# Accumulator copies at the block borders of the second MLP moved ahead of the next step's polynomial, and the last three steps' products with g_l taken last

## The chip, the cores and the metric

The kernel runs on one core of one Trainium2 chip. The metric is the device time of one execution in microseconds (us). A core has five engines with queues of their own: TensorE (PE in the profile; PEld are its weight loads), VectorE (DVE), ScalarE (ACT), GpSimd (POOL) and SyncE (SP), which here only issues DMAs. They meet through semaphores: an instruction adds to one when it is done, and another queue waits until it has a count. Each queue runs strictly in its own order, so whatever stands behind a waiting instruction waits too.

## The reference

A linear attention over 4 batches of 768 positions (8 heads of 48) gives 3072 tokens of 384 numbers. Two MLPs with 2048 hidden features follow:

```python
def _moe_ref(x, w_in, w_out):
    h = x @ w_in
    r = np.maximum(h, 0.0)
    return (r * r) @ w_out

def _moe2_ref(x, w_in, w_out):
    h = x @ w_in
    g = h - np.tanh(h)
    return (g @ w_out).astype(np.float32)
```

The change is in the second MLP and in the turn to it from the first.

## The kernel before

**Tiling.** The 3072 tokens are 6 blocks of 512 columns (`BLOCKS`), the 2048 hidden features 16 tiles of 128 (`FT`). A step m is one tile of one block, m = 16 i + f, 96 steps an MLP. For each step TensorE computes a hidden tile of 128 x 512 (`first1`, `first2`) and adds its contribution to three accumulators acc[0], acc[1], acc[2] of 128 x 512 in PSUM (`second1`, `second2`). Each float32 number is split into a rounded high part and a remainder, and each product is three products, high x high, high x low and low x high (`product3`, lines 542 to 544; the traces call the data `_h` and `_l`). So either half of a step is nine matmuls of 512 columns, a step eighteen.

**Order on TensorE.** Hidden tiles run three steps ahead (`LAG = 3`): first2(m + 3), second2(m), first2(m + 4), second2(m + 1), and so on. In the last three steps no hidden tile is left. Hidden tiles lie in four PSUM buffers in turn, named sc and hid in the traces. When a block ends (f = 15), its accumulators must be copied out before second2 of the next block may start again on them: it waits for ScalarE's copies of acc[0] and acc[2] (semaphore s_outa) and VectorE's copy of acc[1] (s_outd), each just ahead of the products that need it.

**From a hidden tile to g.** g = h - tanh(h) is computed with a short polynomial where h is small. For step k, in this order:
- ScalarE squares the tile (`square`, line 424), shifts the square (`shifted`, line 430), and puts the table's tanh into PSUM, tile y (`table_tanh`, line 434).
- POOL multiplies the shifted square by the square (`square_poly`, line 340).
- ScalarE makes the ratio of it (`make_ratio`, line 438).
- VectorE in `poly_pick(k)` compares the square with a bound (line 820), multiplies tile and ratio (line 822), picks the table's tanh where the square is large (line 826), and subtracts (line 831), which gives g_f.
- ScalarE rounds g_f to g_h (`hi2`, line 445), and POOL takes the remainder g_l (`lo2`, line 345). second2(k) waits for g_l.

ScalarE's order for a step is that of `step2(k)`: square(k), shifted(k), table_tanh(k), hi2(k-1), make_ratio(k). POOL's is square_poly(k), lo2(k-1). At a block border (m = 16 i + 15, k = m + 3) the copies come in: on ScalarE acc[0] and acc[2] around table_tanh(k), with the copies on line 463, and on VectorE acc[1] (`keep_out`, line 840) behind poly_pick(k). SyncE stores each copied accumulator to the output (line 297), three stores of 256 KB a block, the last three at the very end.

**The turn between the MLPs.** The first three hidden tiles of the second MLP and their step2 run in the last three steps of the first. The first MLP's last accumulators are copied by `keep_x2(5)`: on ScalarE lines 417 and 419, behind step2(2); on VectorE line 767, ahead of poly_pick(2). Behind its copies ScalarE converts the last unit of the second MLP's weights (`split_hi`, line 392), and POOL takes that unit's remainder (`split_lo`, line 335) ahead of square_poly(3). `split_x2` (ScalarE line 455, VectorE line 835) splits the next block's input in steps 4 to 6 of each block.

Of the kernel before, what the change touches and what calls it, by code (L numbers as in the profile page):

```python
# [9 lines left out]
ACT = mybir.ActivationFunctionType  # L10
AX_X = mybir.AxisListType.X

P = 128
# [3 lines left out]
KC, FT = C // P, FF // P  # L17
# [7 lines left out]
STEPS = BLOCKS * FT  # L25
LAG = 3
# [13 lines left out]
def build(nc, tt, nat, w_col, u_rep, win1, wout1, win2, wout2, out):  # L40
    with ExitStack() as ctx:
# [11 lines left out]
        wout_h = sb("wout_h", [P, FT, C], F32R)  # L53
        wout_l = sb("wout_l", [P, FT, C], F32R)

        x2T = sb("x2T", [P, BLOCKS, KC, N])
# [4 lines left out]
        g_h = sb("g_h", [P, 4, N], F32R)  # L61
        g_l = sb("g_l", [P, 4, N], F32R)
# [45 lines left out]
        acc = [acc01[:, 0:512], acc01[:, 512:1024], acc2[:, :]]  # L108
# [279 lines left out]
        @block.scalar  # L388
        def _(act):
            def split_hi(mlp, n):  # L390
                act.wait_ge(*landed(mlp, n))
                act.activation(unit_parts(n)[0], unit_raw(mlp, n), ACT.Copy).then_inc(s_whi, 1)

            def diagonal(T):

                act.wait_ge(s_c, T + 1)
                after(act, s_y, T - 1)
                for h in range(H):
                    ins = act.activation(scores[T % 2][:, h % 2, h // 2, :], ident, ACT.Copy,  # L399
                                         scale=c_sum[T % 2][:, h:h + 1])  # L400
                ins.then_inc(s_diag, 1)

            def x_high(T):
                i, j = T // TPB, T % TPB
                act.wait_ge(s_y, T + 1)
                after(act, s_h1, FT * (i - 1))
                act.activation(x_h[:, i % 2, :, P * j:P * j + P],
                               y_ps(T)[:, 0:KC * P].rearrange("p (c t) -> p c t", c=KC), ACT.Copy).then_inc(s_xh, 1)

            def hi1(m):  # L410
                act.wait_ge(s_g1, m + 1)
                after(act, s_o1, m - 3)
                act.activation(g_h[:, m % 4, :], g_f[:, m % 2, :], ACT.Copy).then_inc(s_gh1, 1)  # L413

            def keep_x2(i):
                act.wait_ge(s_acc1, 2 * i + 1)
                act.activation(x2T[:, i, 0, :], acc[0], ACT.Copy).then_inc(s_x2a, 1)
                act.wait_ge(s_o1, FT * i + FT)
                act.activation(x2T[:, i, 2, :], acc[2], ACT.Copy).then_inc(s_x2a, 1)

            def square(m):
                act.wait_ge(s_h2, m + 1)
                after(act, s_sel, m - 1)
                act.activation(sq[m % 2], hid2[m % 4], ACT.Square).then_inc(s_sq, 1)

            def shifted(m):

                act.wait_ge(s_sq, m + 1)
                after(act, s_small, m - 1)
                act.activation(ratio[m % 2], sq[m % 2], ACT.Copy, bias=C3_OVER_C5).then_inc(s_qq, 1)  # L430

            def table_tanh(m):
                after(act, s_sel, m)
                act.activation(tanh_ps[:, :], hid2[m % 4], ACT.Tanh).then_inc(s_tanh, 1)

            def make_ratio(m):
                act.wait_ge(s_pp, m + 1)
                act.activation(ratio[m % 2], ratio[m % 2], ACT.Copy, scale=C5, bias=1.0).then_inc(s_ratio, 1)  # L438

            def hi2(m):  # L440
                act.wait_ge(s_g2, m + 1)
                if m < 4:
                    act.wait_ge(s_o1, STEPS - 3 + m)
                after(act, s_o2, m - 3)
                act.activation(g_h[:, m % 4, :], g_f[:, m % 2, :], ACT.Copy).then_inc(s_gh2, 1)  # L445

            def split_x2(i, c):

                act.wait_ge(s_x2a, 2 * i + 2)
                act.wait_ge(s_x2d, i + 1)  # L450
                if i < 2:
                    act.wait_ge(s_h1, STEPS - FT * (1 - i))
                else:
                    act.wait_ge(s_h2, FT * (i - 1))
                act.activation(x_h[:, i % 2, c, :], x2T[:, i, c, :], ACT.Copy).then_inc(s_x2h, 1)

            def keep_out(i, c):
                if c == 0:
                    act.wait_ge(s_acc2, 2 * i + 1)
                else:  # L460
                    act.wait_ge(s_o2, FT * i + FT)
                after(act, s_x2l, KC * (i + 1))
                act.activation(x2T[:, i, c, :], acc[c], ACT.Copy).then_inc(s_outa, 1)

            act.wait_ge(s_powT, 1)
            act.activation(dec_k, hid34[:, 0:512].rearrange("p (h e) -> p h e", h=H)[:, :, 0:D],
                           ACT.Copy).then_inc(s_tab, 1)
            act.wait_ge(s_const, 3)
            diagonal(0)
            diagonal(1)  # L470
            split_hi(0, 0)
            x_high(0)
            diagonal(2)
            x_high(1)
            diagonal(3)
            x_high(2)
            split_hi(0, 1)
            x_high(3)
            split_hi(0, 2)
            for m in range(LAG):  # L480
                hi1(m)

            def step2(k, ends=None):

                if k < STEPS:
                    square(k)
                    shifted(k)
                if ends is not None:
                    keep_out(ends, 0)
                if k < STEPS:  # L490
                    table_tanh(k)
                if ends is not None:
                    keep_out(ends, 2)
                if k > 0:
                    hi2(k - 1)
                if k < STEPS:
                    make_ratio(k)

            for i in range(BLOCKS):
                for n in range(FT):  # L500
                    m = FT * i + n
                    T = scores_at(i, n)
                    if T is not None:
                        diagonal(T)
                    if m + LAG < STEPS:
                        hi1(m + LAG)
                    T = y_at(i, n)
                    if T is not None:
                        x_high(T)
                    if i == 0 and n in SPLIT1_AT:  # L510
                        split_hi(0, SPLIT1_AT[n])
                    if i == BLOCKS - 1 and n in SPLIT2_AT:
                        u = SPLIT2_AT[n]
                        if u % 2 == 0:
                            act.wait_ge(s_h1, STEPS - FT + 2 * u + Q)
                        else:
                            act.wait_ge(s_o1, STEPS - FT + 2 * (u - 1) + Q)
                        split_hi(1, u)
                    if i == BLOCKS - 1 and n in SPLIT_X2_AT:
                        split_x2(0, SPLIT_X2_AT[n])  # L520
                    if m + LAG >= STEPS:
                        step2(m + LAG - STEPS)
                    if n == FT - 1:
                        keep_x2(i)
            act.wait_ge(s_o1, STEPS)
            split_hi(1, SPLIT2_AT[FT])
            for m in range(STEPS):
                i, n = divmod(m, FT)
                k = m + LAG
                if k <= STEPS:  # L530
                    step2(k, i if n == FT - 1 else None)
                elif n == FT - 1:
                    keep_out(i, 0)
                    keep_out(i, 2)
                if n in SPLIT_X2_AT and i < BLOCKS - 1:
                    split_x2(i + 1, SPLIT_X2_AT[n])

        @block.tensor
        def _(pe):
# [92 lines left out]
            def first2(m):  # L632
# [11 lines left out]
                                  x_h[:, i % 2, c, :], x_l[:, i % 2, c, :], c == 0, c == KC - 1)  # L644
                mm.then_inc(s_h2, 1)

            def second2(m):
                i, f = divmod(m, FT)
                pe.wait_ge(s_gl2, m + 1)
# [46 lines left out]
            for m in range(STEPS):  # L696
                if m + LAG < STEPS:
                    first2(m + LAG)
                second2(m)

        @block.vector
        def _(dve):
# [62 lines left out]
            def keep_x2(i):  # L765
                dve.wait_ge(s_acc1, 2 * i + 2)
                dve.tensor_copy(x2T[:, i, 1, :], acc[1]).then_inc(s_x2d, 1)
# [70 lines left out]
            def keep_out(i):  # L838
                dve.wait_ge(s_acc2, 2 * i + 2)
                dve.tensor_copy(x2T[:, i, 1, :], acc[1]).then_inc(s_outd, 1)  # L840
# [27 lines left out]
                        poly_pick(m + LAG - STEPS)  # L868
            for m in range(STEPS):
                i, n = divmod(m, FT)  # L870
                if m + LAG < STEPS:
                    poly_pick(m + LAG)
                if n in SPLIT_X2_AT and i < BLOCKS - 1:
                    split_x2(i + 1, SPLIT_X2_AT[n])
                if n == FT - 1:
                    keep_out(i)


def feature_order():
# [62 lines left out]
```

## Time and profile before

| | |
|---|---|
| median of 3 runs | 936.95 us (936.81 to 939.05) |
| the profiled execution | 937.0 us, its span 935.2 us |
| TensorE's mean granted clock | 0.983 |
| busy share of the span: PE, PEld, DVE, ACT, POOL | 96%, 79%, 63%, 48%, 51% |
| chain that ended last | PE 80%, DVE 8%, ACT 4%, POOL 3%, issue 3%, DMA 1% |
| turn to the second MLP | about 530 us from the span's start |

Times in the rows count from the start of the span, in us. The profiled execution's time beside its span, 937.0 and 935.2, differs by 1.8 us, which lie around the span. Ends of matmuls are modelled: a matmul's row lasts 0.39 us, while the next one starts 0.227 us later. The granted clock is a share of TensorE's full speed of 2.4 GHz; 0.50 is the lower level, 1.2 GHz. A row's name in brackets is the instruction whose end released it, and the number ahead of it the idle time of the engine before the row.

### The profile page before, as it was taken

To read this page: it belongs to the slowest core of one execution; us is meant where nothing else is said; L and a number is where in the kernel's file an instruction comes from. 1 tells how busy PE (TensorE), PEld (TensorE's weight loads), DVE (VectorE), ACT (ScalarE), POOL (GpSimd) and SP (SyncE) were. 2 spreads that over 40 slices of the span, in tenths; PEclk is the share of its full clock that TensorE was granted. 3 is DMA by queue.
4 is the path that set the end of the run, shared out by engine and by line. 5 is a ranking of instruction groups with operands and counts; after the bars stand their busy time and mean duration, and the time that the engine had idled before them with its cause. 6 is when DMAs were issued, how large, how long until landed. Compare 5 with 4: busy or idle time off the path is not lost.

```text
span 935.2 us, 13868 instructions
## 1 busy us (share of the span) xinstructions
PE 901.3 (96%) x5340; PEld 739.3 (79%) x5340; DVE 589.1 (63%) x789; ACT 453.5 (48%) x852; POOL 479.9 (51%) x370
## 2 busy tenths in 40 slices
PE   5889999999999999999999999999999999999998
PEld 5767888888888888888888788788788788788786
DVE  6368645545554554454356587687687687687675
ACT  3333413222321322232223677677677677677674
POOL 5444344425334432433346777566566566566564
PEclk8799999999999999999999999999999999999999
DMA  6343111210211121120113000000000000000000
GB/s 250 129 180 138 53 52 53 105 53 21 84 53 53 53 105 53 29 78 25 78 61 108 1 1 1 34 1 1 34 0 1 34 1 1 34 1 1 35 0 34
DMA packets 12162, 47.49 MB, mean 51 GB/s; under 512 B 1472, under 2 KB 1600, under 8 KB 12096
## 3 DMA queue, kind: packets, MB, share of 16 engines
q1 hardware_dynamic: 12096, 46.60, 13.6%
q8 instruction: 42, 0.69, 0.3%
q14 instruction: 24, 0.20, 0.1%
HBM read 41.88 MB, written 4.72 MB: 50 GB/s over the span
## 4 chain that ended last, share of the span: by engine, by line
PE 80%; DVE 8%; ACT 4%; issue 3%; POOL 3%; DMA 1%; POOLq 0%; DVEq 0%; ACTq 0%
PE acc L542 13%; PE acc L544 12%; PE acc L543 12%; PE hid L543 9%; PE hid L544 9%; PE hid L542 9%; PE sc L542 3%; PE sc L543 3%; PE sc L544 3%; PE sc L560 3%; PE y L588 2%; PE sc L596 2%; PE y L574 2%; POOL area L340 1%; POOL g_l L345 1%
## 5 line engine op out<-in xcount | busy, mean ns | idle before, releaser
L329 POOL TENSOR_TENSOR g_l<-g_f,g_h 128x512 fp32r<-128x512 f32 x96 | 131.6, 1372 | 277.4 <-ACT g_h L413 277.4
L542 PE MATMUL acc<-g_h,wout_h 128*128 128x512 f32 x576 | 230.3, 400 | 13.1 <-DVE x2T L840 10.1
L544 PE MATMUL acc<-g_h,wout_l 128*128 128x512 f32 x576 | 225.8, 392 | 0.0
L543 PE MATMUL acc<-g_l,wout_h 128*128 128x512 f32 x576 | 225.2, 391 | 0.0
L413 ACT ACTIVATE g_h<-g_f 128x512 fp32r<-128x512 f32 x96 | 60.7, 632 | 315.9 <-DVE g_f L763 299.4
L340 POOL TENSOR_TENSOR area<-area 128x512 f32<-128x512 f32 x96 | 125.6, 1309 | 120.7 <-ACT area L430 120.7
L761 DVE TENSOR_SCALAR g_f<-hid 128x512 f32<-128x512 f32 x96 | 66.2, 690 | 164.4 <-PE hid L544 161.4
L542 PE MATMUL hid<-x_h,win_h 128*128 128x512 f32 x432 | 168.4, 390 | 1.4 <-DVE g_f L761 1.4
L543 PE MATMUL hid<-x_l,win_h 128*128 128x512 f32 x432 | 168.1, 389 | 0.0
L544 PE MATMUL hid<-x_h,win_l 128*128 128x512 f32 x432 | 168.0, 389 | 0.0
L345 POOL TENSOR_TENSOR g_l<-g_f,g_h 128x512 fp32r<-128x512 f32 x96 | 131.2, 1366 | 28.0 <-ACT g_h L445 27.8
L542 PEld LDWEIGHTS acc<-g_h,wout_h 128*128 128x128 f32 x576 | 108.7, 189 | 40.8 <-issue 15.2
L820 DVE TENSOR_SCALAR area<-area 128x512 f32<-128x512 f32 x96 | 83.0, 864 | 71.8 <-POOL area L340 71.2
L544 PEld LDWEIGHTS acc<-g_h,wout_l 128*128 128x128 f32 x576 | 108.7, 189 | 23.2
L543 PEld LDWEIGHTS acc<-g_l,wout_h 128*128 128x128 f32 x576 | 108.8, 189 | 21.3
L542 PEld LDWEIGHTS hid<-x_h,win_h 128*128 128x128 f32 x432 | 81.1, 188 | 18.9 <-DVE g_f L761 2.0
L543 PEld LDWEIGHTS hid<-x_l,win_h 128*128 128x128 f32 x432 | 81.1, 188 | 16.9
L544 PEld LDWEIGHTS hid<-x_h,win_l 128*128 128x128 f32 x432 | 81.1, 188 | 16.9
L826 DVE COPY_PREDICATED area<-area,y 128x512 f32<-128x512 uint32 x96 | 71.5, 745 | 3.3
L763 DVE TENSOR_TENSOR g_f<-g_f 128x512 f32<-128x512 f32 x96 | 70.9, 738 | 3.3
L399 ACT ACTIVATE area<-area,x2T 128x128 f32<-128x128 f32 x192 | 58.8, 389 | 28.2 <-DVE x2T L720 28.2
L438 ACT ACTIVATE area<-area 128x512 f32<-128x512 f32 x96 | 60.0, 625 | 19.3 <-POOL area L340 19.1
(105 smaller groups left out, 1163.6 us busy)
## 6 DMA issues: line engine op xcount, KB each, us to landing
x2T<-in_nat SPq DMA_DIRECT2D x13, 672.0 KB, 5.1
area<-in_nat SPq DMA_DIRECT2D x11, 672.0 KB, 5.0
x2T<-in_tt SPq DMA_DIRECT2D x12, 512.0 KB, 3.8
area<-in_tt SPq DMA_DIRECT2D x11, 512.0 KB, 3.6
out<-x2T SPq DMA_DIRECT2D x18, 256.0 KB, 2.1
x2T<-in_win SPq DMA_DIRECT2D x4, 768.0 KB, 7.8
x2T<-in_wout SPq DMA_DIRECT2D x4, 768.0 KB, 5.0
area<-in_win SPq DMA_DIRECT2D x4, 768.0 KB, 4.2
```

Source lines behind the costliest of these rows:

```text
L329: pool.tensor_tensor(g_l[:, m % 4, :], g_f[:, m % 2, :], g_h[:, m % 4, :].bitcast(F32), ALU.subtract).then_inc(s_gl1, 1)
L340: pool.tensor_tensor(ratio[m % 2], ratio[m % 2], sq[m % 2], ALU.mult).then_inc(s_pp, 1)
L345: pool.tensor_tensor(g_l[:, m % 4, :], g_f[:, m % 2, :], g_h[:, m % 4, :].bitcast(F32), ALU.subtract).then_inc(s_gl2, 1)
L413: act.activation(g_h[:, m % 4, :], g_f[:, m % 2, :], ACT.Copy).then_inc(s_gh1, 1)
L438: act.activation(ratio[m % 2], ratio[m % 2], ACT.Copy, scale=C5, bias=1.0).then_inc(s_ratio, 1)
L542: pe.matmul(dst, wh, xh, start=first, stop=False)
L543: pe.matmul(dst, wh, xl, start=False, stop=False)
L544: return pe.matmul(dst, wl, xh, start=False, stop=last)
L761: dve.tensor_scalar(g, hid1[m % 2], 0.0, None, ALU.max).then_inc(s_relu, 1)
L763: dve.tensor_tensor(g, g, g, ALU.mult).then_inc(s_g1, 1)
L820: dve.tensor_scalar(sq[m % 2], sq[m % 2], Q_SMALL, None, ALU.is_ge).then_inc(s_big, 1)
L826: dve.copy_predicated(tanh[m % 2], sq[m % 2].bitcast(U32), tanh_ps[:, :]).then_inc(s_sel, 1)
```

## The change

Three edits. In the second MLP's block borders, ScalarE's `step2` makes the ratio of step k right behind the two accumulator copies and the g_h copy of step k-1 after it, where the ratio was last; VectorE's `keep_out` stands ahead of `poly_pick(m + 3)` instead of behind it. At the turn, ScalarE's `keep_x2(5)` becomes part of step2(2) in the same manner, instead of standing behind it. In the last three steps of TensorE `second2_low_last` takes the place of `second2`: it waits for g_h, does the six products with g_h, waits for g_l, and does the three products with g_l. `keep_x2` now takes the accumulator's number; for the other blocks its two copies stand where they stood.

```diff
@@ scalar
-            def keep_x2(i):
-                act.wait_ge(s_acc1, 2 * i + 1)
-                act.activation(x2T[:, i, 0, :], acc[0], ACT.Copy).then_inc(s_x2a, 1)
-                act.wait_ge(s_o1, FT * i + FT)
-                act.activation(x2T[:, i, 2, :], acc[2], ACT.Copy).then_inc(s_x2a, 1)
+            def keep_x2(i, c):
+                if c == 0:
+                    act.wait_ge(s_acc1, 2 * i + 1)
+                else:
+                    act.wait_ge(s_o1, FT * i + FT)
+                act.activation(x2T[:, i, c, :], acc[c], ACT.Copy).then_inc(s_x2a, 1)
...
-            def step2(k, ends=None):
+            def step2(k, keep=None, ends=0):
                 if k < STEPS:
                     square(k)
                     shifted(k)
-                if ends is not None:
-                    keep_out(ends, 0)
+                if keep is not None:
+                    keep(ends, 0)
                 if k < STEPS:
                     table_tanh(k)
-                if ends is not None:
-                    keep_out(ends, 2)
+                if keep is not None:
+                    keep(ends, 2)
+                    if k < STEPS:
+                        make_ratio(k)
                 if k > 0:
                     hi2(k - 1)
-                if k < STEPS:
+                if k < STEPS and keep is None:
                     make_ratio(k)
...
-                    if m + LAG >= STEPS:
+                    if m == STEPS - 1:
+                        step2(LAG - 1, keep_x2, i)
+                    elif m + LAG >= STEPS:
                         step2(m + LAG - STEPS)
-                    if n == FT - 1:
-                        keep_x2(i)
+                    elif n == FT - 1:
+                        keep_x2(i, 0)
+                        keep_x2(i, 2)
...
                 if k <= STEPS:
-                    step2(k, i if n == FT - 1 else None)
+                    if n == FT - 1:
+                        step2(k, keep_out, i)
+                    else:
+                        step2(k)
@@ tensor
+            def second2_low_last(m):
+                f = m % FT
+                pe.wait_ge(s_gh2, m + 1)
+                for c in range(KC):
+                    cs = slice(P * c, P * c + P)
+                    pe.matmul(acc[c], wout_h[:, f, cs], g_h[:, m % 4, :], start=False, stop=False)
+                    pe.matmul(acc[c], wout_l[:, f, cs], g_h[:, m % 4, :], start=False, stop=False)
+                pe.wait_ge(s_gl2, m + 1)
+                for c in range(KC):
+                    mm = pe.matmul(acc[c], wout_h[:, f, P * c:P * c + P], g_l[:, m % 4, :],
+                                   start=False, stop=(f == FT - 1))
+                    if f == FT - 1 and c < KC - 1:
+                        mm.then_inc(s_acc2, 1)
+                mm.then_inc(s_o2, 1)
...
             for m in range(STEPS):
                 if m + LAG < STEPS:
                     first2(m + LAG)
-                second2(m)
+                    second2(m)
+                else:
+                    second2_low_last(m)
@@ vector
             for m in range(STEPS):
                 i, n = divmod(m, FT)
+                if n == FT - 1:
+                    keep_out(i)
                 if m + LAG < STEPS:
                     poly_pick(m + LAG)
                 if n in SPLIT_X2_AT and i < BLOCKS - 1:
                     split_x2(i + 1, SPLIT_X2_AT[n])
-                if n == FT - 1:
-                    keep_out(i)
```

## Rows read from the trace of the kernel before

**Rows 1.** Waits of PE over the whole span: us in total, times, longest

```profile
PE acc L542 <- DVE x2T L840: 10.1, 5, 2.0
...
PE acc L542 <- ACT x2T L417: 1.7, 1, 1.7
...
PE acc L542 <- POOL g_l L345: 1.3, 2, 1.0
```

**Rows 2.** Stretches of 4 us behind two borders, with granted clock, DMA share, GB/s

```profile
600.00:604.00 4.00, 4.00 (x11) 3.16 (x12) 2.49 (x4) 0.57 (x1) 1.50 (x1) 0.57 0.35 131
...
804.00:808.00 4.00, 3.76 (x10) 3.04 (x11) 2.64 (x5) 0.79 (x2) 1.74 (x2) 0.60 0.35 131
```

**Rows 3.** Timeline at the first border of the second MLP: start, us, what

```profile
593.22 0.60 ACT L424 ACTIVATE area<-hid 128x512 f32<-128x512 f32 x1 [0.78 <-PE hid L544]
...
594.56 1.29 POOL L340 TENSOR_TENSOR area<-area 128x512 f32<-128x512 f32 x1 [1.53 <-ACT area L430]
...
594.72 0.69 DVE L831 TENSOR_TENSOR g_f<-sc,area 128x512 f32<-128x512 f32 x1
...
595.86 0.63 ACT L445 ACTIVATE g_h<-g_f 128x512 fp32r<-128x512 f32 x1
...
596.38 0.63 ACT L438 ACTIVATE area<-area 128x512 f32<-128x512 f32 x1
...
596.57 1.30 POOL L345 TENSOR_TENSOR g_l<-g_f,g_h 128x512 fp32r<-128x512 f32 x1 [0.71 <-ACT g_h L445]
...
597.56 0.39 PE L544 MATMUL acc<-g_h,wout_l 128*128 128x512 f32 x1
...
599.14 0.68 DVE L840 COPY x2T<-acc 128x512 f32<-128x512 f32 x1
...
599.97 0.72 PE L542 MATMUL acc<-g_h,wout_h 128*128 128x512 f32 x1 [2.02 <-DVE x2T L840]
```

**Rows 4.** Timeline of ACT: squaring of the last two steps, 94 and 95

```profile
917.95 0.60 ACT L424 ACTIVATE area<-hid 128x512 f32<-128x512 f32 x1 [0.71 <-PE hid L544]
...
922.03 0.60 ACT L424 ACTIVATE area<-hid 128x512 f32<-128x512 f32 x1 [0.78 <-PE hid L544]
```

**Rows 5.** Timelines at the turn, of PE, ACT, DVE and POOL

```profile
531.66 0.47 PE L542 MATMUL acc<-g_h,wout_h 128*128 128x512 f32 x1 [1.67 <-ACT x2T L417]
...
543.99 0.46 PE L542 MATMUL acc<-g_h,wout_h 128*128 128x512 f32 x1
...
531.89 1.49 ACT L392 ACTIVATE wout_h<-area 128x1536 fp32r<-128x1536 f32 x1
...
529.77 0.68 DVE L767 COPY x2T<-acc 128x512 f32<-128x512 f32 x1
...
528.84 1.29 POOL L340 TENSOR_TENSOR area<-area 128x512 f32<-128x512 f32 x1 [0.37 <-ACT area L430]
...
533.46 3.50 POOL L335 TENSOR_TENSOR wout_l<-area,wout_h 128x1536 fp32r<-128x1536 f32 x1 [1.55 <-ACT wout_h L392]
...
538.17 1.29 POOL L345 TENSOR_TENSOR g_l<-g_f,g_h 128x512 fp32r<-128x512 f32 x1
...
542.59 1.30 POOL L345 TENSOR_TENSOR g_l<-g_f,g_h 128x512 fp32r<-128x512 f32 x1 [1.20 <-ACT g_h L445]
```

**Rows 6.** Timeline of DVE and PE in the last steps, and a stretch of the last stores

```profile
873.40 0.43 DVE L820 TENSOR_SCALAR area<-area 128x512 f32<-128x512 f32 x1
...
920.62 1.50 DVE L820 TENSOR_SCALAR area<-area 128x512 f32<-128x512 f32 x1 [1.14 <-POOL area L340]
...
923.52 0.69 DVE L831 TENSOR_TENSOR g_f<-hid,area 128x512 f32<-128x512 f32 x1
...
926.93 0.69 DVE L831 TENSOR_TENSOR g_f<-hid,area 128x512 f32<-128x512 f32 x1
...
929.69 0.50 PE L542 MATMUL acc<-g_h,wout_h 128*128 128x512 f32 x1 [1.03 <-POOL g_l L345]
...
933.20:934.00 0.80, 0.00 (x0) 0.00 (x0) 0.00 (x0) 0.00 (x0) 0.00 (x0) 1.00 1.02 379
```

## The prediction

> **What bounds the kernel now.** I read the waits of TensorE first. Over the whole span its longest item in the second MLP is 10.1 us in five waits, the longest 2.0, for the vector engine's copy on line 840 [rows 1]. That is the copy of acc[1] in keep_out, once at each of the five borders between two blocks. Beside it stand one wait of 1.7 us for ScalarE's copy on line 417 (the turn from the first MLP to the second) and 1.3 us in two waits for g_l at the very end [rows 1]. Everywhere else TensorE runs without a pause: ScalarE squares two neighbouring hidden tiles 4.08 us apart (917.95 and 922.03) [rows 4], which is 18 products, or 0.227 us each. So in this stage TensorE sets the time, and the other three engines matter only where TensorE waits for them.
>
> Next, the stretches of the granted clock: 600 to 604 shows 0.57 and 11 products, 804 to 808 shows 0.60 and 10 [rows 2], where 17.6 would fit. These stretches follow two of the five waits, and most of each ran at the lower level, 1.2 GHz. The missing 6.6 and 7.6 products, at 0.227 us, are 1.5 and 1.7 us. So a border can cost more than its wait.
>
> The true cost of the borders needs no counting of single gaps. Step 18 is squared at 593.22 [rows 3] and step 95 at 922.03 [rows 4]. Undisturbed, 77 steps would take 77 x 4.08 = 314.16 us; they took 328.81. **The excess is 14.65 us**: 10.1 of waits, about 3.2 of the two clock drops, the rest restarts.
>
> **Why a border waits.** Take the first, m = 15 [rows 3]. ScalarE squares the hidden tile of step 18 at 593.22, shifts it, makes two accumulator copies and a tanh, then the g_h copy of step 17 (line 445, 595.86), and only then the ratio of step 18 (line 438, 596.38). VectorE needs that ratio: it has ended step 17 at 594.72 + 0.69 = 595.41, but then stands in front of step 18's polynomial, and its copy of acc[1] starts only behind that, at 599.14. TensorE had begun the last product of acc[0] of step 16 at 597.56, would have begun acc[1] at 597.79, and begins at 599.97, after 2.02 us of idling for that copy [rows 3].
>
> **Part 1, VectorE's copy first.** The product of 597.56 is the 21st since step 15's accumulator products began, so these began at 597.56 - 20 x 0.227 = 593.02. acc[1] is complete with the sixth, at 593.02 + 5 x 0.227 + 0.39 = 594.55. VectorE is free at 595.41. The copy then ends at 595.41 + 0.68 = 596.1, 1.7 us before 597.79: the wait is gone. What the copy delays: the comparison of step 18 needs POOL's product of 594.56 + 1.29 = 595.85 anyway, so it starts 0.2 us later and takes 0.43 when POOL is idle (line 820 at 873.40 [rows 6]); it ends as the ratio does, at 596.5.
>
> **Part 2, ScalarE's order at a border.** The ratio moves ahead of the g_h copy of step 17. It needs POOL's 595.85, and ScalarE is free for it from 595.86, when it began the g_h copy. So it starts at 595.9 instead of 596.38; the g_h copy starts 0.52 behind it (the distance of 596.38 from 595.86), at 596.42 instead of 595.86, 0.56 later. Behind it stands POOL's g_l of step 17, which started at 596.57 and now starts near 597.13, ending at 598.4. TensorE began step 16's accumulator products at 597.11 (two products before 597.56) and with the wait gone begins step 17's 4.08 later, at 601.2: 2.8 us of cover. Its next customer on POOL, the product of step 19, follows the squaring of step 19 at 593.22 + 4.08 = 597.3 by 594.56 - 593.22 = 1.34, so it starts at 598.64 and isn't delayed. No DMA is moved; the stores of acc[1] only go out earlier.
>
> With no wait there is no pause in TensorE at the border, and I count the clock drops as gone with it. The trace has the drop right behind the pause at both places and none in a stretch of the second MLP without a pause. The Trainium skill's page "TensorE: Matmul & The Clock Gate" (Why this matters for your kernels) warns only of idle gaps longer than these. By that rule the drops have another cause and 3.2 us would stay, so that the borders would give 11.4; this trace has them behind gaps of 2.0 us all the same. Parts 1 and 2: **-14.65 us**.
>
> **Part 3, the turn between the MLPs** [rows 5]. keep_x2 of the last block now sits inside step2(2). TensorE idled 1.67 and began at 531.66. Its rows show products of 0.39 that follow each other by 0.227, so it could have begun 1.67 + 0.16 = 1.83 earlier, at 529.83. Both copies can now be made before the ratio, and VectorE's own copy (already ahead of the polynomial) ended at 529.77 + 0.68 = 530.45, just when acc[1] would be wanted, at 529.83 + 3 x 0.227 = 530.51. So the wait goes. But what is late next is POOL. It has a 3.50 us subtraction for the last weight unit, begun at 533.46 behind ScalarE's conversion at 531.89, and then owes the product of step 3, g_l of step 2 (538.17 to 539.46) and g_l of step 3 (542.59 + 1.30 = 543.89, against TensorE's 543.99). The conversion can come earlier only as far as ScalarE gets there: the ratio of step 2 waits for POOL's 528.84 + 1.29 = 530.13, then the g_h copy, then the conversion, each 0.53 behind the one ahead: 530.17 + 2 x 0.53 = 531.23 instead of 531.89. So POOL's chain moves 0.65 us, and TensorE, having won 1.83, gives back 0.9 at step 2 (g_l at 538.8, wanted at 529.83 + 2 x 4.08 = 538.0) and 0.3 at step 3 (g_l at 543.24). Net **-0.65 us**, bounds 0 and -1.83.
>
> **Part 4, the last three steps** [rows 6]. Eighteen of the 27 products now start on g_h alone and the nine with g_l follow; the number of products and of weight loads is the same. Of TensorE's 1.3 us of waits for g_l [rows 1] 1.03 stand before step 95, whose products began at 929.69. The chain ahead of it: last subtraction on VectorE 926.93 + 0.69 = 927.62, g_h 0.04 + 0.63 later at 928.29, then POOL's g_l of some 1.3. With the same chain, TensorE (free at 929.69 - 1.03 - 0.16 - 0.42, the last being the older small wait and its restart, 928.0) would begin the first six near 928.35 and the last three 1.5 later, at 929.8: the accumulators would be complete at 930.6 instead of 929.69 + 9 x 0.23 + 0.3 = 932.0.
>
> The chain ahead does not stay the same. Steps alternate: where POOL's g_l product starts first, VectorE's comparison on line 820 takes 1.50 us (920.62, step 94), where not, 0.43 (873.40, step 83). From the squaring to the start of the last subtraction step 94 took 923.52 - 917.95 = 5.57 and step 95 took 926.93 - 922.03 = 4.90 [rows 4, 6]. At the last of the five borders the stall broke the alternation: 82 and then 83, with its comparison at 873.40 right behind the late copy, were both quick, and from there the even steps were slow. Without the stall POOL's g_l of step 82 is ready to start with step 83's product done, so 83 is slow, 84 quick, and so on: 95 becomes a slow one, and its g_h and g_l come 0.67 later, at 928.96 and 930.3. Then the first six products start near 929.0, the last three at 930.5, and TensorE ends at 931.3 instead of 932.0. What is late next is the store: three transfers of 256 KB. The DMA engines moved 379 GB/s at a share of 1.02 in 933.2 to 934.0 [rows 6]: they are full, 0.69 us a transfer. acc[0] was complete with the third product of step 95, at 929.69 + 0.5 + 0.4 = 930.6; now it is with the seventh, at 930.5 + 0.4 = 930.9. From its copy on the three stores run back to back, and end where they did or 0.3 later; before, they had a gap of some 0.1 to 0.2. So part 4 with the slow step 95: **0.0 us**; bounds +0.3 (the first store later) and -0.6 (quick step 95, everything 0.67 earlier, the first store 0.4 earlier than before).
>
> The Trainium skill's page "DMA: Bandwidth & Descriptors" (the table of the two cost components) gives a transfer a fixed cost of about 2.0 us plus its bytes. Applied to the last store alone, issued some 0.6 earlier, the end would come 0.6 earlier; the full engines in the trace speak against it.
>
> **Sum:** 14.65 + 0.65 + 0.0 = 15.3 us. The profiled execution took 937.0 (span 935.2), 0.05 above the median of 936.95; 937.0 - 15.3 = **921.7 us**.
>
> **Rivals.**
> *The clock drops stay*, for a reason other than the pause: 3.2 us more, 924.9. For it: the cause isn't shown by five gaps of which three had no drop. Against: the two drops of the second MLP both stand behind a pause. 0.12. This is also what the rule of "TensorE: Matmul & The Clock Gate" of the Trainium skill would make of it.
> *The turn or the end gives its full due*: 1.2 more at the turn, 0.6 at the end, or both: 919.9 to 921.1. Against: POOL's 3.50 us block, the full DMA engines. 0.15.
> *Another wait takes half of each border*: if VectorE is held at the head of its queue by acc[1] or the polynomial comes late, g of steps 17 and 18 is late. 1 us and more of each 2.0 stays, perhaps with its clock drop: 929. Against: the covers of 1.7 and 2.8 us above. 0.07.
> *Slower*: the g_h copy behind the ratio makes g_l of step 17 late. At each border TensorE would wait for line 345 instead of line 840. It begins to cost from 2.8 us of delay on, and 0.56 is worked out. To end 2.8 us over the time before, it must take back the 15.3 too: 18.1 / 5 = 3.6 us a border, a delay of 6.4 us; the time is then 939.8. 0.02.
> *The change does nothing*, because another copy (ScalarE's on line 463) held TensorE all the time: 937. The waits name line 840 five times of five. 0.02.
> *The forecast* 0.62.
>
> **How the numbers follow.** The likeliest is 921.7. The range takes in the full turn and quick end (919.9) at the low side and the clock rival (924.9) with a late store at the high side: 919.5 to 925.5; outside lie the half-given borders, the slower and the idle case, 0.11, and a little of what lies between. Faster by over 0.3% (2.8 us, about what a measurement of this kernel can tell from no change): the forecast and all rivals but two, 0.96; within 0.3%: 0.02; slower: 0.02.
>
> **What the profile after would show.** No wait for line 840 among TensorE's; copies on line 840 starting about 2.2 us after the squaring of the step whose polynomial followed, where it was 5.9; 77 steps from 18 to 95 in 314.2 us; no stretch behind step 20 at a clock under 1.00. At the turn, two short waits for g_l of line 345, 0.9 and 0.3. Step 95's comparison 1.50 us, a TensorE wait of about 1 us before the last step, for ScalarE's g_h, and stores ending where they did relative to step 95's squaring. What would make it wrong: a clock drop without a pause; a wait on line 345 or 831 at the borders; the alternation kept as it was.

## The result, and the profile after

| | median | runs | ratio to before, 95% interval |
|---|---|---|---|
| before | 937.64 us | 4 (936.81 to 939.05) | |
| changed | 922.61 us | 4 (921.89 to 923.01) | 0.9835 [0.9823, 0.9846] |

The changed kernel is 15.0 us faster; 921.7 was forecast. Its profiled execution took 922.49 (span 920.7), 14.5 us less than the one before.

The waits of TensorE in the second MLP of the changed kernel, the answer to [rows 1] (line 446 is ScalarE's g_h copy, line 345 POOL's g_l; line 662 is the first product of `second2_low_last`):

```profile
PE acc L662 <- ACT g_h L446: 0.9, 1, 0.9
...
PE acc L551 <- POOL g_l L345: 0.5, 1, 0.5
```

No wait for VectorE's copy is left, nor the one for ScalarE's copy at the turn. The stretches of [rows 2] now hold 19 products each, where they had 11 and 10, and stand at full clock:

```profile
600.00:604.00 4.00, 4.00 (x19) 3.30 (x19) 3.51 (x4) 2.81 (x5) 2.47 (x2) 1.00 0.00 0
804.00:808.00 4.00, 4.00 (x19) 3.30 (x19) 3.51 (x4) 2.81 (x5) 2.47 (x2) 1.00 0.01 2
```

The timeline at the first border of the second MLP, beside [rows 3] (lines 425, 439 and 446 of the changed kernel are the square, the ratio and the g_h copy, 867 is VectorE's copy):

```profile
593.23 0.60 ACT L425 ACTIVATE area<-hid 128x512 f32<-128x512 f32 x1 [0.78 <-PE hid L553]
...
595.90 0.63 ACT L439 ACTIVATE area<-area 128x512 f32<-128x512 f32 x1
596.44 0.62 ACT L446 ACTIVATE g_h<-g_f 128x512 fp32r<-128x512 f32 x1
...
594.74 0.69 DVE L858 TENSOR_TENSOR g_f<-sc,area 128x512 f32<-128x512 f32 x1
595.34 0.68 DVE L867 COPY x2T<-acc 128x512 f32<-128x512 f32 x1
...
597.13 1.30 POOL L345 TENSOR_TENSOR g_l<-g_f,g_h 128x512 fp32r<-128x512 f32 x1 [1.26 <-ACT g_h L446]
```

The square stands at 593.23, as before at 593.22, so the rows compare directly. VectorE copies at 595.34 instead of 599.14, the ratio comes at 595.90 instead of 596.38, the g_h copy at 596.44 instead of 595.86, and POOL's g_l at 597.13 instead of 596.57. All four were forecast to within 0.1.

The whole time splits at three squarings. From the g_h copy of step 0 to the squaring of step 18 is the turn, from there to the squaring of step 95 are the borders, the rest is the end. The start of the turn is this row in the timeline of the kernel before; behind it stand its like and the squaring of step 95 in the changed kernel:

```profile
526.46 0.63 ACT L445 ACTIVATE g_h<-g_f 128x512 fp32r<-128x512 f32 x1
```
```profile
527.10 0.63 ACT L446 ACTIVATE g_h<-g_f 128x512 fp32r<-128x512 f32 x1
...
907.39 0.60 ACT L425 ACTIVATE area<-hid 128x512 f32<-128x512 f32 x1 [0.70 <-PE hid L553]
```

| stretch | before | changed | difference | forecast |
|---|---|---|---|---|
| start to g_h copy of step 0 | 526.46 | 527.10 | +0.64 | none |
| turn | 66.76 | 66.13 | -0.63 | -0.65 |
| steps 18 to 95 | 328.81 | 314.16 | -14.65 | -14.65 |
| step 95 to the end of the span | 13.17 | 13.31 | +0.14 | 0.0 |
| sum | 935.2 | 920.7 | -14.5 | -15.3 |

The first row isn't touched by the change. It read 524.66 to 527.40 over the profiles of this study: 527.10 and 526.81 in two of the changed kernel, whose spans were 920.7 and 920.4.

### The profile page after: what moved, and what is told of

It reads as the page before. It is cut to its first block, busy times and chain, and to the rows that moved or that the text cites. A ratio compares the mean times of both kernels' runs of the same rounds, so it can differ in the third digit from the quotient of the medians.

```text
span 920.7 us, 13868 instructions
## 1 busy us (share of the span) xinstructions
PE 896.6 (97%) x5340; PEld 736.9 (80%) x5340; DVE 591.2 (64%) x789; ACT 453.1 (49%) x852; POOL 477.1 (52%) x370
## 4 chain that ended last, share of the span: by engine, by line
PE 82%; DVE 8%; POOL 4%; ACT 3%; issue 2%; DMA 1%; ACTq 0%; DVEq 0%; POOLq 0%
PE acc L551 13%; PE acc L553 12%; PE acc L552 12%; PE hid L551 9%; PE hid L552 9%; PE hid L553 9%; PE sc L552 3%; PE sc L553 3%; PE sc L551 3%; PE sc L569 2%; PE y L597 2%; PE sc L605 2%; PE y L583 2%; POOL area L340 1%; DVE area L847 1%
## 5 line engine op out<-in xcount | busy, mean ns | idle before, releaser
L329 POOL TENSOR_TENSOR g_l<-g_f,g_h 128x512 fp32r<-128x512 f32 x96 | 131.6, 1372 | 278.1 <-ACT g_h L413 278.1
L551 PE MATMUL acc<-g_h,wout_h 128*128 128x512 f32 x567 | 225.8, 398 | 0.6 <-POOL g_l L345 0.5
L553 PE MATMUL acc<-g_h,wout_l 128*128 128x512 f32 x567 | 221.9, 391 | 0.0
L552 PE MATMUL acc<-g_l,wout_h 128*128 128x512 f32 x567 | 221.4, 391 | 0.0
L345 POOL TENSOR_TENSOR g_l<-g_f,g_h 128x512 fp32r<-128x512 f32 x96 | 128.4, 1338 | 33.6 <-ACT g_h L446 33.6
L551 PEld LDWEIGHTS acc<-g_h,wout_h 128*128 128x128 f32 x567 | 106.7, 188 | 25.8 <-POOL g_l L345 1.5
L847 DVE TENSOR_SCALAR area<-area 128x512 f32<-128x512 f32 x96 | 88.3, 920 | 59.3 <-POOL area L340 59.3
L553 PEld LDWEIGHTS acc<-g_h,wout_l 128*128 128x128 f32 x567 | 106.8, 188 | 22.8
L552 PEld LDWEIGHTS acc<-g_l,wout_h 128*128 128x128 f32 x567 | 106.8, 188 | 21.0
```

The source lines that it names most:

```text
L329: pool.tensor_tensor(g_l[:, m % 4, :], g_f[:, m % 2, :], g_h[:, m % 4, :].bitcast(F32), ALU.subtract).then_inc(s_gl1, 1)
L345: pool.tensor_tensor(g_l[:, m % 4, :], g_f[:, m % 2, :], g_h[:, m % 4, :].bitcast(F32), ALU.subtract).then_inc(s_gl2, 1)
L551: pe.matmul(dst, wh, xh, start=first, stop=False)
L552: pe.matmul(dst, wh, xl, start=False, stop=False)
L553: return pe.matmul(dst, wl, xh, start=False, stop=last)
L847: dve.tensor_scalar(sq[m % 2], sq[m % 2], Q_SMALL, None, ALU.is_ge).then_inc(s_big, 1)
```

## The experiments

The span is quoted in the same stretches. "Turn" and "end" are those of the table. Stretches are read from one profiled execution each, ratios from all runs.

**VectorE's edit alone.** The kernel before, with

```diff
+                if n == FT - 1:
+                    keep_out(i)
                 if m + LAG < STEPS:
                     poly_pick(m + LAG)
...
-                if n == FT - 1:
-                    keep_out(i)
```

> The kernel before with only VectorE's edit: its copy of acc[1] ahead of the polynomial. My theory: the five waits and the clock drops behind them hang on this copy alone, and ScalarE's order only shortens a chain that has cover. Steps 18 to 95 then take 314.2 us instead of 328.8, and nothing else moves by more than 0.7: 922.3 to 923.1 us in a run whose first MLP is like that of the profile before (14.0 to 14.7 less than the kernel before). Rival: ScalarE's order is needed too, since the ratio of the border's step stays 0.48 later; then TensorE waits for a g_l one or two steps behind the border, and the gain is half, some 7 us.

922.02 us, 0.9828 [0.9814, 0.9843] of the kernel before, which is the changed kernel's figure within both intervals. Step 18 was squared at 592.96 and step 95 at 907.12: 314.16 us. The turn stayed 66.76. Its end is 13.18, and its last steps hold a surprise (line 820 is the comparison):

```profile
907.12 0.60 ACT L424 ACTIVATE area<-hid 128x512 f32<-128x512 f32 x1 [0.78 <-PE hid L544]
...
909.79 0.43 DVE L820 TENSOR_SCALAR area<-area 128x512 f32<-128x512 f32 x1 [0.48 <-POOL area L340]
```

TensorE has no wait at any border, and step 95 is still a quick one: its comparison takes 0.43. The prediction had made the missing stall the reason for a slow one.

**ScalarE's order alone.** The changed kernel with VectorE's loop and the last three steps of the kernel before:

```diff
-                if n == FT - 1:
-                    keep_out(i)
                 if m + LAG < STEPS:
                     poly_pick(m + LAG)
...
+                if n == FT - 1:
+                    keep_out(i)
...
-                    second2_low_last(m)
+                    second2(m)
```

> The changed kernel with VectorE's order and the last three steps put back: only ScalarE's order at the borders and at the turn is new. My theory: the ratio comes 0.48 us earlier, so VectorE's late copy does, and the pause at each border shrinks from 2.0 to about 1.5 us: 5 x 0.48 = 2.4 us, with 0.65 at the turn, 3.0 us less than before; with fewer clock drops up to 3.2 more. 931 to 934.5 us. Rival: the ratio's place is what removes the wait, then the five waits are gone here too and the time is that of the changed kernel, 922.6.

930.95 us, 0.9922 [0.9907, 0.9937]. All five waits are there, 0.46 us shorter each, with no fall of the clock behind any; the first of them, and their sum:

```profile
599.77 0.47 PE L551 MATMUL acc<-g_h,wout_h 128*128 128x512 f32 x1 [1.55 <-DVE x2T L867]
```
```profile
PE acc L551 <- DVE x2T L867: 7.8, 5, 1.6
```

Steps 18 to 95 took 916.76 - 593.50 = 323.26 us, 5.55 less than before: 5 x 0.46 = 2.3 from the waits and 3.2 from the two falls of the clock that are missing here. The turn took 66.10, 0.66 less. The ratio's place alone doesn't remove the wait. Step 95 is quick here, with the new order and the stall:

```profile
919.43 0.43 DVE L847 TENSOR_SCALAR area<-area 128x512 f32<-128x512 f32 x1 [0.48 <-POOL area L340]
```

**The old last steps.** The changed kernel with

```diff
-                    second2_low_last(m)
+                    second2(m)
```

> The changed kernel with the old order of the products in the last three steps (step 95 is a slow one). My theory: TensorE waits for g_l of step 95 until about 1.3 us later than it now waits for g_h, then runs nine products instead of three; the first store starts 0.4 to 0.7 later, and from the squaring of step 95 to the end of the span there are 13.7 to 14.0 us instead of 13.31. Rival: the three products taken last give the whole 1.3 us, then it is 14.6. Other rival: the stores hide all of it, 13.3.

923.60 us in one run. The end is 921.8 - 906.51 = 15.3 us, more than any theory said. The wait, and the stretch of the clock around it:

```profile
914.83 0.79 PE L551 MATMUL acc<-g_h,wout_h 128*128 128x512 f32 x1 [2.02 <-POOL g_l L345]
```
```profile
914.00:916.00 2.00, 1.17 (x3) 0.97 (x4) 0.00 (x0) 0.00 (x0) 0.78 (x1) 0.71 0.00 0
```

TensorE pauses 2.02 us and goes on at the lower level. From its first product to the copy of acc[2] it took 918.78 - 914.83 = 3.95 us, where the run with VectorE's edit alone, at full clock, took 917.16 - 914.79 = 2.37. Without these 1.58 the end would be 13.7, at the lower edge of the first theory; no run shows this order with a slow step 95 and no fall.

**A longer pause at the borders.** The kernel before with the copy of acc[1] made twice, and in another run three times (with a loop around the added lines):

```diff
             def keep_out(i):
                 dve.wait_ge(s_acc2, 2 * i + 2)
+                if i < BLOCKS - 1:
+                    dve.tensor_copy(x2T[:, i, 1, :], acc[1]).then_inc(s_extra, 1)
+                    dve.wait_ge(s_extra, i + 1)
                 dve.tensor_copy(x2T[:, i, 1, :], acc[1]).then_inc(s_outd, 1)
```

> The kernel before with VectorE's copy of acc[1] made twice at each of the five borders, so that TensorE's pause grows from 2.0 to about 2.75 us. Both theories: 5 x 0.75 = 3.7 us more. If the clock falls because of the pause, a longer pause makes it fall more often: three to five of the five borders show a stretch at the lower level, 1.6 us each, and the time is 5.4 to 8.6 us over the kernel before. If the falls have a cause of their own, there are about two as before, and it is 3.7 us more.

> The kernel before with VectorE's copy of acc[1] made three times at each of the five borders: a pause of some 3.5 us each, 7.5 us more of waits than in the kernel before. With pauses of 2.0 us two of five borders had a fall of the clock, with 2.8 one of five, with 2.6 two of five, with 1.6 none. If length decides once it is long enough, four or five of five fall here. If it is when a pause comes that decides, any number from none to five, and again the same answer at borders that lie equally far apart.

With two copies: 938.79 us in the median of 10 runs, 1.0003 [0.9993, 1.0012]. The waits had grown as meant, by 3.6 us in all, and the time had not:

```profile
PE acc L542 <- DVE x2T L843: 13.7, 5, 2.8
```
```profile
602.00:604.00 2.00, 2.00 (x6) 1.61 (x5) 1.35 (x2) 0.00 (x0) 0.00 (x0) 0.50 0.29 110
670.00:672.00 2.00, 1.63 (x7) 1.40 (x8) 1.97 (x4) 0.25 (x1) 0.92 (x1) 1.00 0.46 171
```

One border of five has a fall here (602 to 604 at 0.50), the second (670 to 672 at 1.00) has none. The other three have none either, so its profile has one fall where the kernel before has two, and its steps 18 to 95 take 330.87 us, 2.06 more. The medians point the same way: 3.6 us more of waits and 0.3 us more of time. The longer pause brought fewer falls, not more, and both theories failed. (The mean granted clock of its runs, 0.987 to 0.991 against 0.981 to 0.987 for the kernel before beside it, isn't a count of these falls: in the two profiles most of that difference lies in the first 60 us, at 0.87 and 0.81.)

The medians also allow a rough estimate of how many falls a typical execution of the kernel before has. Beside VectorE's edit alone it took 938.5, 16.5 us more than that run; the waits and restarts of its profile are 14.65 less the 3.2 of two falls, 11.4. The 5.1 left are about three falls of 1.6. Beside ScalarE's order alone 7.6 us lie between the medians, of which the waits and the turn are 3.0; the 4.6 left are three again. Its profiled execution, with two, took 936.95.

With three copies, 952.71 us in one run, pauses of 3.47 us, and a fall behind every one:

```profile
602.00:604.00 2.00, 1.87 (x5) 1.52 (x6) 1.93 (x4) 0.00 (x0) 0.00 (x0) 0.50 0.58 218
674.00:676.00 2.00, 2.00 (x6) 1.51 (x6) 0.94 (x2) 0.00 (x0) 0.00 (x0) 0.50 0.41 154
744.00:746.00 2.00, 2.00 (x6) 1.53 (x5) 1.53 (x3) 0.00 (x0) 0.00 (x0) 0.50 0.73 262
816.00:818.00 2.00, 2.00 (x6) 1.52 (x5) 1.13 (x2) 0.00 (x0) 0.00 (x0) 0.50 0.53 193
888.00:890.00 2.00, 2.00 (x6) 1.60 (x5) 0.78 (x2) 0.00 (x0) 0.00 (x0) 0.50 0.32 120
```

**g_l of the border's step late on purpose.** The changed kernel, in which POOL makes g_l of step 17 (and of its like at the other four borders) three times, and in another run five times:

```diff
+                if k % FT == LAG - 1 and k > LAG:
+                    pool.wait_ge(s_gh2, k)
+                    after(pool, s_o2, k - 4)
+                    for x in range(2):
+                        pool.tensor_tensor(g_l[:, (k - 1) % 4, :], g_f[:, (k - 1) % 2, :],
+                                           g_h[:, (k - 1) % 4, :].bitcast(F32), ALU.subtract).then_inc(s_extra, 1)
+                        pool.wait_ge(s_extra, 2 * (k // FT - 1) + x + 1)
                 lo2(k - 1)
```

> The changed kernel in which POOL makes the g_l of the step in front of each border's polynomial three times instead of once, at the five borders: some 2.7 us later. This stands at the edge of the 2.8 us of cover that was worked out less the 0.56 that ScalarE's order took. My theory: g_l of step 17 then ends at about 601.1, TensorE wants it at 601.2: no wait or one of 0.1 to 0.3 us a border, so 0 to 1.5 us over the changed kernel. Rival: there is less cover than worked out (the queue behind it, the product of step 19, is what TensorE waits for); then 1 us and more a border, 5 us and more in all.

> As the run with three, but five times instead of once: some 5.4 us later, 2.6 over the cover. My theory: each border now costs a wait of 2.4 to 2.8 us for g_l on line 345, five of them, and what comes with a pause of that length: 12 to 14 us over the changed kernel without clock drops, up to 8 more with them. This is the rival that was called slower, made to happen. Rival: the cover is larger than worked out, and nothing or half of it is seen.

Three times: 922.6 us, 0.9832 [0.9816, 0.9849], no difference from the changed kernel that can be measured. In the trace steps 18 to 95 take 1.1 us more, 0.2 a border, and the end takes 12.98 us, 0.3 less, as step 95 is a quick one here. Five times: 936.91 in one run, 14.3 us over the changed kernel's 922.61. Its wait at the first border, and the waits in total (0.5 of them at the turn):

```profile
601.63 0.50 PE L558 MATMUL acc<-g_h,wout_h 128*128 128x512 f32 x1 [2.57 <-POOL g_l L345]
```
```profile
PE acc L558 <- POOL g_l L345: 13.4, 6, 2.6
```

The cover was sized right: 2.7 us of delay cost 0.2, 5.4 us cost 2.6. Of these five pauses, two had a fall of the clock.

**Step 95 made quick.** The changed kernel with

```diff
+                if k == STEPS - 1:
+                    pool.wait_ge(s_big, k + 1)
                 lo2(k - 1)
```

> The changed kernel, in which POOL's g_l of step 94 waits for VectorE's comparison of step 95, so that this comparison should take 0.43 instead of 1.50 us. My theory: step 95 becomes a quick one, g_h and g_l of it come 0.67 us earlier, g_l of step 94 comes 0.5 later and is not missed (TensorE takes it last), and the first store starts 0.6 earlier: from the squaring of step 95 to the end of the span 12.6 to 12.8 us instead of 13.31. Rival: the alternation has nothing to do with the comparison's neighbour on POOL, then 13.3.

921.26 us in one run. The end is 919.5 - 906.87 = 12.6 us. POOL idles while VectorE makes the comparison of step 95, which takes 0.43, and TensorE's wait of 0.9 shrinks to 0.18:

```profile
909.54 0.43 DVE L849 TENSOR_SCALAR area<-area 128x512 f32<-128x512 f32 x1 [1.14 <-POOL area L340]
...
913.13 0.50 PE L664 MATMUL acc<-g_h,wout_h 128*128 128x512 f32 x1 [0.18 <-ACT g_h L448]
```

**The ratio back in its old place.** The changed kernel with ScalarE's old order at the five borders, the new one at the turn:

```diff
-                    if k < STEPS:
+                    if k < LAG:
                         make_ratio(k)
                 if k > 0:
                     hi2(k - 1)
-                if k < STEPS and keep is None:
+                if k < STEPS and (keep is None or k >= LAG):
                     make_ratio(k)
```

> The changed kernel with ScalarE's old order (the g_h copy, then the ratio) at the five borders; at the turn the new order stays. The run with VectorE's edit alone had step 95 quick although its borders had no stall, so the reason given in the prediction for the slow step 95 (the stall gone) can't be the whole. New theory: it is ScalarE's order, which lets g_l of the border's step be ready in front of the next comparison. Then step 95 is quick here, its comparison 0.43 us, the end 12.6 to 13.0 us behind its squaring, and the borders still have no wait: 0.4 to 0.7 us less than the changed kernel. Theory of the prediction: the stall alone decides, then step 95 is slow here, 13.3.

920.0 us in one run. No wait at a border, 314.16 us from step 18 to 95, and step 95 quick: its comparison took 0.43, the end 918.2 - 905.55 = 12.65 us. So the missing stall alone doesn't make step 95 slow; in the changed kernel it takes ScalarE's order too.

**The last weight unit later.** The changed kernel with

```diff
-            act.wait_ge(s_o1, STEPS)
-            split_hi(1, SPLIT2_AT[FT])
             for m in range(STEPS):
                 i, n = divmod(m, FT)
+                if m == 8:
+                    act.wait_ge(s_o1, STEPS)
+                    split_hi(1, SPLIT2_AT[FT])
...
-            split_lo(1, SPLIT2_AT[FT])
             for k in range(LAG, STEPS + 1):
                 if k < STEPS:
                     square_poly(k)
                 lo2(k - 1)
+                if k == 10:
+                    split_lo(1, SPLIT2_AT[FT])
```

> The changed kernel with the last weight unit of the second MLP converted by ScalarE in step 8 instead of ahead of step 0, and its remainder taken by POOL behind g_l of step 9 instead of ahead of step 3 (it is first used in step 12). My theory: at the turn POOL's chain is what is late; without the 3.50 us block the two waits of 0.9 and 0.3 us that were forecast there (0.55 and about 0.2 in the profile) go, the turn gives 0.8 to 1.2 us more, and TensorE doesn't wait for POOL in steps 9 to 12, where g_l has 2.8 us of cover against 3.5 of block less POOL's idle time of 1.5 a step. From ScalarE's g_h copy of step 0 to the squaring of step 18: 66.13 us in the changed kernel, 65.0 to 65.4 here. Rival: another wait takes its place (the block is only moved, and TensorE waits as long for g_l of step 10), then 66.1.

920.23 us, 0.9807 [0.9792, 0.9821]. The turn is 590.95 - 526.06 = 64.89 us, 1.24 less, and no wait for POOL is left in the second MLP.

**Both together, beside the changed kernel.**

> The changed kernel with the last weight unit moved to step 8 and POOL's g_l of step 94 behind VectorE's comparison of step 95. The two gains were 1.24 us at the turn and 0.68 at the end when made alone. They lie at two ends of the stage, so they should add: 1.9 us less than the changed kernel run beside it. In the trace: 64.9 us from ScalarE's g_h copy of step 0 to the squaring of step 18, 12.6 to 13.0 from the squaring of step 95 to the end of the span, 314.2 between.

> The changed kernel itself, to stand beside the combined one on the same chip: 922 to 923 us, no fall of the clock in the second MLP, 13.3 us from the squaring of step 95 to the end of the span.

The combination took 919.54 us (918.13 to 920.03, 4 runs), 0.9801 [0.9788, 0.9815] of the kernel before; the changed kernel on the same chip 921.36 (921.12 to 922.15, 5 runs), 0.9823 [0.9809, 0.9836]. The runs of the two don't overlap, 1.8 us lie between the medians, 1.9 were expected. Turn 64.94, borders 314.16, end 12.54. It has the lowest median of the study, though its interval overlaps that of the last weight unit alone (0.9807). The changed kernel came out 0.6 us under the 922 to 923 expected, with no fall in the second MLP and an end of 13.33.

## Why the prediction held, point by point

- **The excess of 14.65 us at the borders** was right to the hundredth, for the profiled execution it was read from; one with a fall more or less would have 1.6 us more or less. Reading it as the time of 77 steps against 77 times the distance of two undisturbed ones spared the sum of waits, restarts and clock drops. VectorE's edit alone gives all of it. The parts are 10.1 of waits, 3.2 of two falls, and some 0.26 a border behind each wait: ScalarE's order alone has waits of 7.8, no fall and an excess of 9.1. The prediction's products missing behind a fall were counted against 17.6, where the view counts 19 in an undisturbed stretch. The size was right all the same: in the kernel before, TensorE's first products behind the first three waits stand at 599.97, 669.12 and 736.67, so the block behind a fall took 69.15 us and the next, without one, 67.55.
- **The covers at the border** were right: both the copy at 595.3 and the 2.8 us behind the moved g_h copy, which the runs with three and five g_l bracket. (The rival "slower" counted these 2.8 from the old place of g_l, but they were worked out behind the 0.56 that it moves.)
- **The clock drops gone with the pause**: right for the changed kernel, where TensorE runs at full clock through the whole second MLP. That the pause is the cause is supported: over all profiles, the falls among TensorE's products in the second MLP stand only behind pauses of 2.0 us and more, and none behind the 0.2 to 1.7 us ones. The page "TensorE: Matmul & The Clock Gate" of the Trainium skill (Why this matters for your kernels) warns only of longer gaps. The falls behind 2.02 us here don't agree with it. What decides whether a pause of 2.0 to 2.8 us has a fall stays open: length alone doesn't, since 2.8 us had fewer falls than 2.0.
- **The turn, 0.65 instead of 1.83**: right, 0.63. POOL's 3.50 us block was what came next, at step 2 as forecast. The wait list has it as 0.55, not 0.9, but the list counts from the modelled end of the product ahead. By its start, step 2's first product (539.46) stands 0.94 behind the one ahead of it instead of 0.227, and the product behind it another 0.11 late: 0.8. Step 3's first, 543.90, stands 0.45 behind, with 0.11 more again: 0.3, as forecast, though the list has no wait for it. Some 0.1 more goes at acc[1], as VectorE's copy ends beside the moment it is wanted:

```profile
530.92 0.39 PE L553 MATMUL acc<-g_h,wout_l 128*128 128x512 f32 x1
531.14 0.50 PE L551 MATMUL acc<-g_h,wout_h 128*128 128x512 f32 x1
531.48 0.40 PE L552 MATMUL acc<-g_l,wout_h 128*128 128x512 f32 x1
...
539.46 0.50 PE L551 MATMUL acc<-g_h,wout_h 128*128 128x512 f32 x1 [0.55 <-POOL g_l L345]
...
543.90 0.50 PE L551 MATMUL acc<-g_h,wout_h 128*128 128x512 f32 x1
```

  Moving the block gave the rest, 1.24.
- **The end, 0.0**: right in size, +0.14. Step 95 was slow as forecast, TensorE waited 0.90 for g_h, and the stores ran with the DMA engines full, at a share of 1.03. The three issues take from 916.92 to 918.23, where they took from 931.31 to 933.01. Counted from the squaring of step 95, the first is 0.25 later than before, the last 0.14 sooner, and the end 0.14 later. The page "DMA: Bandwidth & Descriptors" of the Trainium skill (Anatomy of one DMA, the two cost components) gives one transfer that GpSimd issues a fixed cost of about 2.0 us plus its bytes. Taken from the last issue on, that would have put the end 0.14 sooner; the trace doesn't bear it out for these three stores in a row, which SyncE issues. The rows:

```profile
910.06 1.50 DVE L847 TENSOR_SCALAR area<-area 128x512 f32<-128x512 f32 x1 [1.14 <-POOL area L340]
...
914.37 0.50 PE L662 MATMUL acc<-g_h,wout_h 128*128 128x512 f32 x1 [0.90 <-ACT g_h L446]
```
```profile
918.00:919.00 1.00, 0.00 (x0) 0.00 (x0) 0.00 (x0) 0.00 (x0) 0.00 (x0) 1.00 1.03 385
```

- **The reason given for the slow step 95 was half wrong.** "Without the stall ... 83 is slow" named the stall; the runs with VectorE's edit alone and with the old ratio order have no stall and a quick step 95. ScalarE's order alone has the stall and a quick one as well. It takes both: no stall and the ratio ahead of the g_h copy. Even then step 95 is quick when g_l of the border's step comes 2.7 us late, as the run with three g_l has it. So ScalarE's edit at the borders brings nothing there and costs 0.66 us at the end (13.31 against 12.65). That is why the end came out even: with a quick step 95 the new last steps bring 0.53 (12.65 against the 13.18 of VectorE's edit alone).
- **Those last steps** are worth more than the 0.0 of the sum tells. That sum set them against the quick step 95 of the kernel before. Against the old order with a slow step 95 they save 2.0 us (15.3 to 13.31), of which 1.6 come from a fall of the clock behind the pause of 2.02 us in that one profile.

The profiled spans differ by 0.8 us less than the 15.3 that was forecast: 0.64 of it lie in the first MLP, which the change doesn't touch, and 0.14 in the end. The medians differ by 15.0.

## What to carry to other kernels

Where one engine sets the pace, measure what a disturbance costs as the distance between two marks many steps apart, less the undisturbed steps; a sum of waits misses what a pause brings behind it. A copy that frees an accumulator belongs ahead of work that has slack, and here it was enough to move it on the one engine that the waits named; the edit on ScalarE at the borders brought nothing and made the last step slow. When a wait goes, ask what is late next: here a 3.5 us block on POOL took two thirds of the gain at the turn, and moving it eight steps later, under a cover already worked out, gave it back.

## What the runs showed that was not expected

A TensorE pause of 2.0 us can be followed by a fall of the clock to 1.2 GHz, which costs another 1.6 us (2.6 behind three of the pauses of 3.5). Falls among TensorE's products in the second MLP, counted over the profiles with such pauses: 1.6 us, 0 of 5; 2.0 us, 2 of 5 and 1 of 1; 2.6 us, 2 of 5; 2.8 us, 1 of 5; 3.5 us, 5 of 5. Lengthening each of five pauses by 0.75 us left the median time as it was; its profile had one fall instead of two, and the waits add more than one fall gives back, so in the median about two fewer must have come (3.6 of waits against 0.3 of time, an estimate). Each share is from one profiled execution and is rough.
